# Exponentials of the downsampled rows taken from the scores' bank, with the shift as bias and the row sums as a second result, tile by tile

## What is computed

```python
batch, n_heads, seq, head_dim = (4, 8, 576, 64)
...
def sm_attn(qq, kk, vv):
    s = scale * np.matmul(qq, kk.transpose(0, 1, 3, 2))
    s = s - np.max(s, axis=-1, keepdims=True)
    a = np.exp(s)
    a = a / (np.sum(a, axis=-1, keepdims=True) + 1e-09)
    return np.matmul(a, vv)
q_d = q.reshape(B, H, Sd, factor, D).mean(axis=3)      # factor 4, Sd = 144
...
out_up = np.repeat(sm_attn(q_d, k_d, v_d), factor, axis=2)
mask = np.abs(pos[:, None] - pos[None, :]) < factor
scores = np.where(mask, scale * np.matmul(q, k.transpose(0, 1, 3, 2)), -1000000000.0)
...
x = out_up + out_local
...
g = x @ w_gate                                          # 2304 x 512 by 512 x 1536
y = (g * (1.0 / (1.0 + np.exp(-g))) * (x @ w_val)) @ w_out
h = np.maximum(y @ w_in, 0.0)                           # 512 x 2048
return (h * h @ w_out2)
```

## Time and profile before

| | |
|---|---|
| median of 3 runs | 935.19 us (934.59 to 935.87) |
| profiled execution | 935.13 us, of which the span is 933.3 |
| PE, DVE, ACT, POOL busy | 98%, 70%, 43%, 24% of the span |
| mean granted TensorE clock | 0.998 of full speed |

### The profile page before, as it was taken

The page is one execution under the profiler, slowest core; times in us unless marked ns, Lnnn a source line. Parts: engine busy times, 40 slices in busy tenths (PEclk is TensorE's granted clock), DMA queues, the critical chain, the costliest instruction groups (busy, mean ns, idle before and its releaser), DMA issues.

```text
span 933.3 us, 17255 instructions
## 1 busy us (share of the span) xinstructions
PE 912.6 (98%) x6764; PEld 879.2 (94%) x6764; DVE 650.1 (70%) x1111; ACT 403.6 (43%) x733; POOL 226.2 (24%) x279
## 2 busy tenths in 40 slices
PE   8899999999999999999999999999999999999998
PEld 5688999898999999999999999999999999999998
DVE  7855655564476757776757699585879676878775
ACT  3654545454346343546344445141535242435331
POOL 5963545343262000422000223000323000302000
PEclk9999999999999999999999999999999999999999
DMA  9933333231241020331211140010332020221422
GB/s 229 272 107 104 104 98 88 80 84 45 79 137 53 17 59 10 102 102 35 99 38 68 47 154 5 1 35 1 102 102 65 4 63 6 80 66 48 136 68 68
DMA packets 70881, 71.38 MB, mean 76 GB/s; under 512 B 27280, under 2 KB 58000, under 8 KB 70800
## 3 DMA queue, kind: packets, MB, share of 16 engines
q1 hardware_dynamic: 68496, 65.55, 23.9%
q10 hardware_dynamic: 2304, 4.72, 1.4%
HBM read 56.10 MB, written 14.16 MB: 75 GB/s over the span
## 4 chain that ended last, share of the span: by engine, by line
PE 79%; DVE 9%; ACT 5%; issue 2%; POOL 2%; SPq 1%; DMA 1%; ACTq 0%; DVEq 0%; POOLq 0%
PE mlp_ps L939 12%; PE mlp_ps L941 11%; PE mlp_ps L940 11%; PE sc L939 5%; PE sc L941 5%; PE sc L940 5%; PE xp L941 4%; PE xp L939 4%; PE xp L940 4%; PE sd L939 2%; PE sd L941 2%; PE sd L940 2%; PE sc L769 2%; PE tr L788 2%; PE tr L939 2%
## 5 line engine op out<-in xcount | busy, mean ns | idle before, releaser
L1319 ACT ACTIVATE wh_hi<-hbuf 128x384 fp32r<-128x384 f32 x144 | 72.4, 524 | 85.8 <-DVE hbuf L1605 61.1
L689 POOL TENSOR_TENSOR w_raw<-w_raw 128x256 f32<-128x256 f32 x16 | 17.1, 1066 | 355.5 <-DMA w_raw<-w_in 355.5
L1613 DVE TENSOR_TENSOR wh_lo<-hbuf,wh_hi 128x384 fp32r<-128x384 f32 x144 | 76.1, 561 | 24.1 <-ACT wh_hi L1319 20.6
L1568 DVE TENSOR_TENSOR ring<-ring_raw,ring 128x768 fp32r<-128x768 f32 x96 | 90.8, 970 | 0.0
L1268 ACT ACTIVATE ring<-ring_raw 128x768 fp32r<-128x768 f32 x96 | 75.3, 836 | 28.9 <-DVE ring_raw L1562 28.6
L939 PE MATMUL mlp_ps<-ring,w_hi 128*128 128x384 f32 x240 | 80.7, 336 | 2.4 <-DVE vbuf L1581 1.9
L941 PE MATMUL mlp_ps<-ring,w_lo 128*128 128x384 f32 x240 | 80.3, 334 | 0.0
L940 PE MATMUL mlp_ps<-ring,w_hi 128*128 128x384 f32 x240 | 80.3, 334 | 0.0
L939 PE MATMUL mlp_ps<-wh_hi,w_hi 128*128 128x384 f32 x216 | 73.3, 339 | 2.6 <-DVE wh_lo L1613 1.5
L940 PE MATMUL mlp_ps<-wh_lo,w_hi 128*128 128x384 f32 x216 | 72.3, 335 | 0.0
L941 PE MATMUL sc<-wh_hi,w_lo 128*128 128x384 f32 x216 | 72.2, 334 | 0.0
(11 more groups left out here) (202 smaller groups left out, 2711.7 us busy)
## 6 DMA issues: line engine op xcount, KB each, us to landing
ring_raw<-x_whole SPq DMA_DIRECT2D x24, 384.0 KB, 3.7
ring_raw<-y_whole SPq DMA_DIRECT2D x24, 384.0 KB, 3.8
qk_sb<-qT SPq DMA_DIRECT2D x16, 288.0 KB, 2.9
qk_sb<-kT SPq DMA_DIRECT2D x16, 288.0 KB, 3.8
v_grp<-v SPq DMA_DIRECT2D x32, 144.0 KB
x_whole<-x_f ACTq DMA_DIRECT2D x16, 288.0 KB, 2.5
y_whole<-ypart SPq DMA_DIRECT2D x3, 1536.0 KB, 5.7
v_win<-v SPq DMA_DIRECT2D x64, 64.0 KB, 2.8
```

Of the source, the lines that this page charges most:

```text
L689: nc.gpsimd.tensor_tensor(block(5), block(7), block(4), ALU.add).then_inc(s_usum[i], 1)
L1319: nc.scalar.activation(hi[:, f, t, :], hbuf[:, e, :], ACT.Copy).then_inc(s_shhi, 1)
L1568: nc.vector.tensor_tensor(ring[:, SLOTS[g][p], 1, :, :], whole(g, p), ring[:, SLOTS[g][p], 0, :, :].bitcast(F32), ALU.subtract).then_inc(s ...
L1613: nc.vector.tensor_tensor(lo[:, f, t, :], hbuf[:, e, :], hi[:, f, t, :].bitcast(F32), ALU.subtract)\
```

## The change

DVE no longer subtracts the row's maximum from the downsampled scores. It makes a `shift_d` out of the three maxima of each partition (128x3), and ACT takes the exponential directly from the scores' bank `sd`, tile by tile, in three instructions, with the tile's shift as bias. Each of them gives the row sum of its tile as a second result (`total_d`), so that the sum over `probs_d` goes from DVE as well. Since ACT now reads the bank `sd`, others that write it wait for ACT: PE's next downsampled scores (L776), and DVE's local normalisation, which writes its sums there; from pair 4 on the latter waits for the exponentials of its own pair. The wait for the turned rows of the pair before, whose `probs_d` is overwritten, moves from DVE to ACT. The places of the functions in each engine's program are the same.

```diff
--- before.py
+++ after.py
@@ -204,6 +204,8 @@
         ident = sb("ident", [P, P])
         max_l = sb("max_l", [P, 2, TJ])
         max_d = sb("max_d", [P, DT])
+        shift_d = sb("shift_d", [P, DT])
+        total_d = sb("total_d", [P, DT])
         credits = sb("credits", [P, 2])
 
         def late(name, shape, offset, dt=F32):
@@ -254,9 +256,8 @@
         s_norml = sem("s_norml")
         s_sd = sem("s_sd")
         s_maxd = sem("s_maxd")
-        s_subd = sem("s_subd")
+        s_shiftd = sem("s_shiftd")
         s_expd = sem("s_expd")
-        s_sumd = sem("s_sumd")
         s_dend = sem("s_dend")
         s_invd = sem("s_invd")
         s_normd = sem("s_normd")
@@ -773,7 +774,7 @@
 
         def pe_scores_ds(pe, i):
             if i > 0:
-                pe.wait_ge(s_subd, i)
+                pe.wait_ge(s_expd, DT * i)
                 pe.wait_ge(s_norml, i)
             if i > PAIRS:
                 pe.wait_ge(s_normd, i)
@@ -1115,9 +1116,15 @@
               .then_inc(s_expl, 1)
 
         def act_exp_ds(a, i):
-            a.wait_ge(s_subd, i + 1)
-            nc.scalar.activation(probs_d[:, :], probs_d[:, :], ACT.Exp, scale=SCALE / FACTOR ** 2)\
-              .then_inc(s_expd, 1)
+
+            a.wait_ge(s_shiftd, i + 1)
+            if i > 0:
+                a.wait_ge(s_turnd, 2 * i)
+                a.wait_ge(s_dend, i)
+            for q in range(DT):
+                cols = slice(DS * q, DS * (q + 1))
+                nc.scalar.activation(probs_d[:, cols], sd[:, cols], ACT.Exp, bias=shift_d[:, q:q + 1],
+                                     scale=SCALE / FACTOR ** 2, accum_out=total_d[:, q:q + 1]).then_inc(s_expd, 1)
 
         def act_move_loc1(a, i):
             a.wait_ge(s_turn1, i + 1)
@@ -1430,6 +1437,9 @@
             total, den, inv = (sums_loc(k) for k in range(3))
             d.wait_ge(s_expl, i + 1)
             d.wait_ge(s_sd, i + 1)
+
+            if i > 0:
+                d.wait_ge(s_expd, DT * (i if i < PAIRS else i + 1))
             nc.vector.tensor_reduce(total, pl, AX.X, ALU.add).then_inc(s_suml, 1)
             d.wait_ge(s_suml, i + 1)
             nc.vector.tensor_scalar(den, total, EPS, 1.0, ALU.add, ALU.mult).then_inc(s_denl, 1)
@@ -1445,19 +1455,16 @@
             nc.vector.tensor_reduce(max_d[:, :], tiles, AX.X, ALU.max).then_inc(s_maxd, 1)
             d.wait_ge(s_maxd, i + 1)
             if i > 0:
-                d.wait_ge(s_turnd, 2 * i)
-            nc.vector.tensor_tensor(probs_d[:, :].rearrange("p (q k) -> p q k", q=DT), tiles,
-                                    max_d[:, :].unsqueeze(2).to_broadcast([P, DT, DS]),
-                                    ALU.subtract).then_inc(s_subd, 1)
+                d.wait_ge(s_expd, DT * i)
+            nc.vector.tensor_scalar(shift_d[:, :], max_d[:, :], -SCALE / FACTOR ** 2, 0.0, ALU.mult, ALU.add)\
+              .then_inc(s_shiftd, 1)
 
         def dve_normalise_ds(d, i):
-            total, den, inv = (sums_ds(i, k) for k in range(3))
+            den, inv = (sums_ds(i, k) for k in range(2))
             pd = probs_d[:, :].rearrange("p (q k) -> p q k", q=DT)
-            d.wait_ge(s_expd, i + 1)
-            nc.vector.tensor_reduce(total, pd, AX.X, ALU.add).then_inc(s_sumd, 1)
-            d.wait_ge(s_sumd, i + 1)
-
-            nc.vector.tensor_scalar(den, total, EPS, float(FACTOR), ALU.add, ALU.mult).then_inc(s_dend, 1)
+            d.wait_ge(s_expd, DT * (i + 1))
+
+            nc.vector.tensor_scalar(den, total_d[:, :], EPS, float(FACTOR), ALU.add, ALU.mult).then_inc(s_dend, 1)
             d.wait_ge(s_dend, i + 1)
             nc.vector.reciprocal(inv, den).then_inc(s_invd, 1)
             d.wait_ge(s_invd, i + 1)
```

## The result

The changed kernel takes 948.34 us in the median of 4 runs (946.85 to 950.59), the kernel before beside it 935.53 (934.59 to 937.03, 4 runs): a ratio of 1.0137, 95% interval 1.0111 to 1.0164. That is 12.8 us slower; the forecast was 10.7 slower, 945.8 with a range of 940 to 951. The profiled execution took 947.35 us, its span is 945.5 where it was 933.3.

The account below looks back on a forecast made before the run. PE, busy for 98% of the span, was taken as the bound. Start-up 3.1, even pairs 5.4, and odd pairs 1.3 and 1.0 gave 10.7 us unrounded on 935.1: 945.8, range 940 to 951.

Parts of the forecast that it names:

- T: Length of a pair's three downsampled exponentials with their sums on ACT: 1.18 us, range ends 0.88 and 1.5.
- Even pairs: Slots of pairs 6, 8, 10, 12, 14: DVE's local sum waits for the exponentials, T-0.10 each, 5.4 us together.
- Odd pairs: Slots of pairs 5 to 15: longer ACT work delays h_lo; 1.3 us at 5 and 15, 1.0 at the others.
- The step for pairs 7, 9, 11 and 13: h_lo comes 0.63 us later against a slack of 0.39: 4 x (0.63-0.39) = 1.0 us.
- which PE's turn can nearly stand: Odd pairs: exponentials end at 95.66 where DVE reached its local sum at 95.14; nothing charged for PE's turn.
- Start-up: Rounds and the chain to pair 4: PE's turn in slot 0 comes at 49.15 instead of 46.04, 3.1 us later.
- unchanged, -1.7 to +1.7: PE's 1.2 GHz stretch from 46 to 50 us, costing 1.7 us, taken as unchanged; worth -1.7 to +1.7.
- DVE's relief: 17 us of DVE work removed over 16 pairs; gain counted in round 4 only, elsewhere zero.
- Cheap tiles: Rival: sums and bias nearly free, T from 0.55 to 0.75, 2.2 to 4 us, near 938.5; chance 0.08.
- serial reads: Rival: reads of the sums serialise wholly, T of 1.5 to 2, 16 to 24 us; chance 0.09.
- The stalls don't add up: Rival: PE's even-pair waits are hidden, only start-up and odd pairs paid, about 940; chance 0.04.
- the low clock would go and make it faster: Rival: low-clock stretch behind slot 0 goes, -1.7 at 46 to 50 us; 933.7 at T = 0.35; chance 0.02.

Follow-up runs that it names:

- the sums by DVE: Changed kernel, but the exponentials give no second result and DVE sums probs_d as before; 945.36 us, ratio 1.0081.
- own sums: Changed kernel, but the local sums of pairs 4 to 15 go into an SBUF tile instead of the scores' bank; 941.35 us, ratio 1.0048.
- the wait alone: Kernel before, with one wait added: from pair 4 on DVE's local normalisation waits for the pair's downsampled exponential; 940.23 us, ratio 1.0039.
- the longer T: Changed kernel with an unused 128x320 copy on ACT ahead of each pair's three exponentials; 957.14 us, ratio 1.0227.
- the maximum in the bank: Changed kernel, but DVE writes the maximum to free columns of the scores' PSUM bank and the shift reads it there; 946.84 us, ratio 1.0105.
- the exponentials first: Changed kernel, but in rounds 0 to 3 ACT does the exponentials ahead of moving the turned local rows; 948.92 us, ratio 1.0133.
- both edits: Changed kernel with the maximum in the scores' bank and, in the rounds, the exponentials ahead of ACT's move of local probabilities; 946.38 us, ratio 1.0099.
- the shift as a product: Changed kernel, but the shift is a tensor_tensor with a constant SBUF tile in place of the tensor_scalar; 948.36 us, ratio 1.0128.

## Why the prediction was right

**T.** Taken at 1.18, measured 1.17 to 1.19. (The prediction names 1.5 as T's upper end, but its range of 940 to 951 was worked out with 1.38.) The right sum is in part luck: its parts were off in opposite directions and made up for each other. The plain tile with a tensor bias is 0.374, not 0.29 (the prediction had 0.1 for the bias only at its upper end); the second instruction for the sum is there, at 0.20, not 0.17; and every neighbour overlaps by about 0.10, the reads too, where I had let only two of them. At pair 10 the three tiles take 1.11, the three reads 0.59, less five overlaps, 0.52: 1.18. The assumption that the sum is a small instruction of its own carried the number. The estimate from the Trainium skill, "ScalarE: Activation LUTs", section "What ACT_TABLE_LOAD costs" (0.40 a tile, T of 1.01 without sums), is to be held against 0.374 a tile and a T of 0.90 with the sums by DVE: the page's 93 ns for a tensor bias are 83 here, against the plain copy of a tile at 0.291 from PSUM.

**Even pairs.** The mechanism, T-0.10 for each of five stalls, was right; the run with own sums took it away, the wait alone in the kernel before brought it in at half the size, and the longer T scaled it with 0.36 for 0.36. The size was 0.7 short in all: I had DVE start 0.04 behind ACT's end, and it starts 0.13 behind it (148.32 to 148.45), which is 0.09 for each pair and 0.45 of the 0.7. The other 0.2 I did not trace. The chain of waits at pair 10 (start, length, what) shows what lies between, the queue's instruction for the added wait:

```profile
148.33 0.03 issue
148.36 0.05 DVEq L1442
148.41 0.04 issue
148.45 0.84 DVE sd L1443
```

The added wait costs an instruction of its own, even once it is met: the kernel before with the wait alone has the same 0.13 at every even pair, and with own sums, without the wait, it is 0.03.

**Odd pairs.** 2.2 against 2.3, but not as written. The step for pairs 7, 9, 11 and 13 let PE's turn stand the new wait and charged 0.24 for h_lo. The trace charges about 0.25 at the turn itself and almost nothing at h_lo. Pair 7 in the kernel before, then in the changed one:

```profile
96.47 0.82 DVE L1439 TENSOR_TENSOR probs_l<-probs_l,sd 128x640 f32<-128x640 f32 x1
97.77 0.60 PE L788 MATMUL tr<-ident,probs_l 128*128 128x128 f32 x4
...
100.89 0.21 ACT L1126 ACTIVATION_READ_ACCUMULATOR probs_d<-sd,shift_d 128x1 f32 x1
101.23 0.83 DVE L1443 TENSOR_REDUCE sd<-probs_l 128x10 f32<-128x640 f32 x1 [0.56 <-ACT probs_d L1126]
102.56 0.82 DVE L1449 TENSOR_TENSOR probs_l<-probs_l,sd 128x640 f32<-128x640 f32 x1
103.44 0.66 PE L789 MATMUL tr<-ident,probs_l 128*128 128x128 f32 x4
```

Before, the product ended 0.48 ahead of the turn, now the turn follows it by 0.06. Here too the 0.13 enters; the sentence "which PE's turn can nearly stand" was the step that failed, by two tenths. At pairs 5 and 15 the prediction charged 0.63 each, and 0.41 and 0.44 were paid: the wait for h_lo grows by 0.57 at pair 5, but 0.20 comes back at PE's next turn of downsampled rows. That shortfall of 0.4 is made up by pair 13, which has 0.35 more than pairs 9 and 11. There DVE's sum starts 0.48 behind ACT's end and not 0.13:

```profile
199.19 0.83 DVE L1443 TENSOR_REDUCE sd<-probs_l 128x10 f32<-128x640 f32 x1 [0.91 <-ACT probs_d L1126]
```

The same 0.48 stands at this pair in the four experiments whose DVE program has the same instructions in the same order up to there (the longer T, the maximum in the bank, the exponentials first, both edits), and not in the two that have the same wait and one more DVE instruction somewhere ahead of it (the shift as a product, the sums by DVE: 0.13 in both). So it goes with the place in DVE's program and is no accident of one execution; what it is stays open. That the odd pairs come to the right sum is luck.

**Start-up.** 3.9 against 3.1. Rounds 2 and 3 were called at 0.81 each and are 0.83:

```profile
31.08 0.22 ACT L1126 ACTIVATION_READ_ACCUMULATOR probs_d<-sd,shift_d 128x1 f32 x1
31.35 0.96 PE L784 MATMUL sd<-k_ds,q_ds 128*64 128x144 f32 x12 [0.76 <-ACT probs_d L1126]
```

The normalised rows of round 4 are 2.34 later (2.24 predicted). In slot 0 the term that was mis-sized is the shift at 0.17:

```profile
45.49 0.52 DVE L1459 TENSOR_SCALAR shift_d<-max_d 128x3 f32<-128x3 f32 x1
46.05 0.38 ACT L1126 ACTIVATE probs_d<-sd,shift_d 128x144 f32<-128x144 f32 x1 [0.63 <-DVE shift_d L1459]
47.03 0.21 ACT L1126 ACTIVATION_READ_ACCUMULATOR probs_d<-sd,shift_d 128x1 f32 x1
47.37 0.83 DVE L1443 TENSOR_REDUCE sd<-probs_l 128x10 f32<-128x640 f32 x1 [1.36 <-ACT probs_d L1126]
```

It took 0.52 beside POOL, 0.35 more; PE's turn came at 49.58 for 49.15, 3.54 later than before for 3.1. With the shift at 0.16 (the maximum in the bank) the turn comes at 49.12, 3.08 later than before: the prediction's chain with its own value for the shift. The low clock was "unchanged, -1.7 to +1.7". The window behind it tells otherwise:

```profile
50.00:54.00 4.00, 4.00 (x50) 3.29 (x49) 0.46 (x1) 0.60 (x1) 2.51 (x4) 0.57 0.33 96
```

Before it was 1.00 here and 0.57 from 46 to 50. In the changed kernel PE is idle for most of the window from 46 to 50 (busy 1.50 of 4 us), so the low clock costs nothing there, and it works at 0.57 in the next. The difference of starts grows from 3.54 at the turn to 4.05 and is 3.85 at 54 us, so the net is 0.3 against the stretch of before: small, and inside the bound.

**DVE's relief.** Taken at nothing except in round 4. DVE's work went down by 12.5 us (17 predicted; the four long shifts are 3 of the difference), with no gain elsewhere. The run that gave the sums back to DVE, its span 3.7 shorter, says it most plainly.

**The rivals.** Cheap tiles and serial reads both fell with T. "The stalls don't add up" fell with the table. That the low clock would go and make it faster fell too: its stretch reaches over both windows, 46 to 50 and 50 to 54 us, where before it was one, and in the run with the longer T further stretches came.

## What to carry to other kernels

Before work is moved from a free engine onto one whose result releases a PSUM bank, list who waits for that bank, and multiply the new length by the number of those waits that end at the bounding engine: here 16 x T decided, not 17 us of relieved DVE. Results that share a bank only for storage (the local sums) make a wait between engines that have no data in common; but when they are moved to SBUF, count the operations whose inputs then all lie there, because each can be held by GpSimd for as long as it works, and can hold GpSimd in turn. Small operations ahead of a stalled engine need a price for their worst row, not their median.

## What the runs showed of the hardware

- A row sum as second result of an ACTIVATE is a further instruction of 0.19 to 0.22 us; overlapping on both sides, it adds 0.09 for a tile (T of 1.18 with three, 0.90 without).
- An ACTIVATE of 128x144 takes 0.374 from PSUM with a tensor bias, 0.308 from SBUF without; one of 128x432 takes 0.606 and 0.548.
- A DVE tensor_scalar of 128x3 from SBUF took 0.17 to 3.24 us, depending on whether GpSimd was at work when it came and for how long it went on; from PSUM 0.160 to 0.161 in 16 of 16. A product of 128x640 with two SBUF inputs took 0.82 or 1.02 to 1.13 by the same rule, and a GpSimd operation that came while such a product was at work took 1.32 to 1.39 instead of 0.79 to 0.81.
- From ACT's end to DVE's start it is 0.13 us where DVE's queue has one more wait to work off, 0.03 where it has not the earlier trace rows.
- Where stalls of PE grew by 0.36 us each, two places that stood at a granted clock of 1.00 had a mean of 0.57 behind the stall, at 1.5 us each.
